# Narrower maxima, six score pieces, and the last two bodies' value products in three fp32r parts

## The reference

```
scores = q @ k.T / 8 - max(cum_i - cum_j, 0)        # cum: running sum of max(s, 0)
attn   = softmax(causal scores)                     # row maximum subtracted
x      = attn @ v, heads side by side               # (4, 576, 512)
h      = relu(x @ w_in); gate = sigmoid(conv3(h)); x1 = (h * gate) @ w_out
u      = x1 + (x1.T @ U @ V).T                      # U: 576 x 32, V: 32 x 576
out    = u + relu(u @ w_ch1) @ w_ch2
```

## Time and profile before

| | |
|---|---|
| median of 3 runs (884.1 to 886.88) | 885.18 us |
| profiled execution | 886.38 us |
| its span, first to last instruction | 884.6 us |
| PE (TensorE) busy | 853.1 us, 96% |
| DVE (VectorE) busy | 463.5 us, 52% |
| ACT (ScalarE) busy | 380.8 us, 43% |
| share of TensorE in the chain that ended last | 80% |
| mean granted TensorE clock | 0.998 |

### The profile page before, as it was taken

The page is one execution under the profiler, slowest core; times in us unless marked ns, Lnnn a source line. Parts: engine busy times, 40 slices in busy tenths (PEclk is TensorE's granted clock), DMA queues, the critical chain, the costliest instruction groups (busy, mean ns, idle before and its releaser), DMA issues.

```text
span 884.6 us, 15745 instructions
## 1 busy us (share of the span) xinstructions
PE 853.1 (96%) x6184; PEld 805.3 (91%) x6184; DVE 463.5 (52%) x976; ACT 380.8 (43%) x717; POOL 50.6 (6%) x106
## 2 busy tenths in 40 slices
PE   4988999989999999999999999999999999999998
PEld 3766889879998999999999999999999999999998
DVE  6787794565547825563445942555323832442222
ACT  3777674663436535553325642544213722121110
POOL 3021000000000000010000000000000000000000
PEclk9999999999999999999999999999999999999999
DMA  5574736726744346444444436325335443364541
GB/s 125 139 188 118 274 107 209 250 59 217 242 159 172 117 156 225 164 140 160 169 158 142 144 106 221 117 83 194 141 128 194 147 160 129 140 236 152 181 153 54
DMA packets 61837, 140.92 MB, mean 159 GB/s; under 512 B 29515, under 2 KB 43851, under 8 KB 49221
## 3 DMA queue, kind: packets, MB, share of 16 engines
q1 hardware_dynamic: 58692, 135.06, 45.7%
q0 software_dynamic: 3072, 4.87, 2.1%
HBM read 109.71 MB, written 30.11 MB: 158 GB/s over the span
## 4 chain that ended last, share of the span: by engine, by line
PE 80%; DVE 7%; issue 4%; ACT 4%; DMA 2%; SPq 1%; POOL 0%; DVEq 0%; ACTq 0%; POOLq 0%
PE psum L1256 22%; PE psum L1258 21%; PE psum L1257 21%; PE psum L1235 7%; PE psum L1180 2%; PE psum L1213 2%; PE psum L1211 2%; DVE work L1018 1%; DVE psum L959 1%; DVE work L1021 1%; PE psum L1193 1%; DMA few_scratch<-few 1%; PE psum L1322 1%; PE psum L1218 1%; ACT work L794 1%
## 5 line engine op out<-in xcount | busy, mean ns | idle before, releaser
L1256 PE MATMUL psum<-uu_hl,ring 128*128 128x288 f32 x512 | 152.9, 299 | 1.8 <-DVE uu_hl L1056 1.2
L1256 PE MATMUL psum<-r_hl,ring 128*128 128x288 f32 x512 | 152.9, 299 | 0.0
L1258 PE MATMUL psum<-r_hl,ring 128*128 128x288 f32 x512 | 151.2, 295 | 0.0
L1257 PE MATMUL psum<-r_hl,ring 128*128 128x288 f32 x512 | 151.1, 295 | 0.0
L1258 PE MATMUL psum<-uu_hl,ring 128*128 128x288 f32 x512 | 150.9, 295 | 0.0
L1257 PE MATMUL psum<-uu_hl,ring 128*128 128x288 f32 x512 | 150.8, 294 | 0.0
L838 ACT ACTIVATE r_hl<-psum 128x288 fp32r<-128x288 f32 x128 | 52.5, 411 | 187.9 <-PE psum L1258 187.8
L1061 DVE SCALAR_TENSOR_TENSOR r_hl<-psum,r_hl 128x288 fp32r<-128x288 f32 x128 | 58.3, 458 | 136.3 <-ACT r_hl L838 136.3
L959 DVE CUSTOM_DVE_ANT_0 psum<-psum,key_late 128x512 f32<-128x512 f32 (+4 forms) x160 | 84.3, 563 | 54.9 <-PE psum L1180 54.7
L1235 PE MATMUL psum<-probs,va 128*65 128x320 f32 (+4 forms) x448 | 109.3, 364 | 3.3 <-ACT probs L733 3.1
L1073 DVE TENSOR_TENSOR u_acc<-psum,u_acc 128x288 f32<-128x288 f32 x96 | 43.7, 457 | 116.2 <-PE psum L1258 116.2
(11 more groups left out here) (103 smaller groups left out, 1621.3 us busy)
## 6 DMA issues: line engine op xcount, KB each, us to landing
ring<-w_scratch SPq DMA_DIRECT2D x74, 1024.0 KB, 4.9
w_scratch<-ring SPq DMA_DIRECT2D x24, 1024.0 KB, 5.9
kq_raw<-in_kq_t SPq DMA_DIRECT2D x32, 288.0 KB, 4.1
stage<-in_w_ch SPq DMA_DIRECT2D x16, 512.0 KB, 5.8
spread_out<-few_scratch POOLq DMA_DIRECT2D x32, 144.0 KB, 3.1
out_t<-u_acc SPq DMA_DIRECT2D x16, 288.0 KB, 3.6
va<-in_v SPq DMA_DIRECT2D x32, 128.0 KB, 2.7
stage<-in_w_out SPq DMA_DIRECT2D x4, 512.0 KB, 5.1
```

The costliest lines, as they stand in the source:

```text
L1256: pe.matmul(o, hi, m_hi, start=start, stop=False)
L1257: pe.matmul(o, hi, m_lo, start=False, stop=False)
L1258: return pe.matmul(o, lo, m_hi, start=False, stop=stop)
```

## The change

- Tiles of query rows are laid from the end: tile 0 has rows 0 to 63, tile t rows 64 + 128 (t - 1) onwards. The widths of the maxima are 64, 192, 320, 448 and 576 instead of 128, 256, 384, 512 and 576. The rounds are {3, 0}, {2, 1}, {4}.
- Key tile 4 has its own 64 rows only, and the pieces of the scores are (1, 128, 576); (2, 256, 576); (0, 256, 576), (3, 384, 576); (0, 0, 256), (4, 512, 576). Each chunk has a mask product. Value products still end at query 256 where their PSUM bank does.
- U is loaded 96 columns wide instead of 128; the small loads come two steps earlier; V's low part is made a step later. The fp32 identity becomes the fp32r one.
- In bodies 2 and 3 (n >= `PARTED` = 16) ScalarE makes each chunk's exponentials twice, as the high part in one fp32r buffer and as fp32, and the values' high part (`values_high`) at step 0; VectorE makes both low parts; TensorE multiplies high x high and high x low values at step c + 1, and low probabilities x high values in `then` of step c + 1. Exponentials of chunk c are in step c, ahead of its items. The heads' evictions there are in `then` of step 4 except for head 7.

```diff
-    CHUNKS = [[(1, SPLIT, S)],
-              [(2, SPLIT, S)],
-              [(0, SPLIT, S), (3, 3 * P, S)],
-              [(4, 4 * P, S), (1, P, SPLIT), (0, 0, SPLIT)]]
+    CHUNKS = [[(1, P, S, 0)],
+              [(2, SPLIT, S, 0)],
+              [(0, SPLIT, S, 0), (3, 3 * P, S, S - SPLIT)],
+              [(0, 0, SPLIT, P // 2), (4, 4 * P, S, 0)]]
-        ROUNDS = [[3], [2, 0], [1, 4]]
+        ROUNDS = [[3, 0], [2, 1], [4]]
-        SMALL_AT = {(0, 4): 0, (1, 4): 1, (2, 2): 2}
+        SMALL_AT = {(0, 4): 0, (1, 2): 1, (2, 0): 2}
+        PARTED = 2 * H
+        def low_behind(h, c):
+            return h < H - 1 or c < NC - 1
+        def chunk_before(n, c, by):
+            m, at = divmod((n - PARTED) * NC + c - by, NC)
+            return (m, at + 1) if m >= 0 else None
...
-                      if any(x[0] in ("turn", "rank", "mix") for x in PLAN[a][GROUPS * h + GROUPS - 1])}
+                      if any(x[0] in ("turn", "rank", "mix") for x in PLAN[a][GROUPS * h + GROUPS - 1]) or a * H + h >= PARTED}
...
+                def exponentials_parted(a, h, c):
+                    n = a * H + h
+                    mm_s.wait(act, n, c + 1)
+                    if chunk_before(n, c, 1):
+                        mm_hi.wait(act, *chunk_before(n, c, 1))
+                        pl_done.wait(act, *chunk_before(n, c, 1))
+                    act.activation(probs_hl[0][:, 0:WIDTH[c]], psum[:, c % 2, 0:WIDTH[c]], ACT.Exp).then_inc(exps.sem, 1)
...
+                    act.activation(probs[:, c % 2, 0:WIDTH[c]], psum[:, c % 2, 0:WIDTH[c]], ACT.Exp).then_inc(whole.sem, 1)
+                def values_high(a, h):
...
+                    act.activation(va_hl[:, :, 0:D], va[i][:, :, 0:D], ACT.Copy).then_inc(vh_done.sem, 1)
...
                     if STEP_BEFORE.get((a, h, g)):
                         follow(STEP_BEFORE[a, h, g][-1])
+                    if a * H + h >= PARTED and g < NC:
+                        exponentials_parted(a, h, g)
...
+                def probabilities_low(a, h, c):
+                    n = a * H + h
+                    whole.wait(dve, n - PARTED, c + 1)
+                    mm_pv.wait(dve, n, c) if c else mm_pv.wait(dve, n - 1)
...
                 def then(a, h, g):
+                    if g < NC and a * H + h >= PARTED:
+                        probabilities_low(a, h, g)
...
+                    value_products(n, c, [(va_hl[:, :, 0:D + 1], probs_hl[0], True),
+                                          (va_hl[:, :, VLOW:VLOW + D], probs_hl[0], False)]).then_inc(mm_hi.sem, 1)
+                def values_of_low(a, h, c):
+                    n = a * H + h
+                    pl_done.wait(pe, n - PARTED, c + 1)
+                    value_products(n, c, [(va_hl[:, :, 0:D + 1], probs_hl[1], False)]).then_inc(mm_pv.sem, 1)
...
+                def then(a, h, g):
+                    if g >= 1 and a * H + h >= PARTED and low_behind(h, g - 1):
+                        values_of_low(a, h, g - 1)
```

More of the change, by code:

```diff
@@ L501, in load_v @@
                         return
-                    mm_pv.wait(sp, n - 2)
+                    mm_pv.wait(sp, n - 2) if n - 2 < PARTED else vl_done.wait(sp, n - 2 - PARTED)
                     of = v[source(a, h)]
@@ L1178, in max_scores @@
                             if r == 2 and n and bank not in started:
-                                red.wait(pe, n, 1 if bank == MX // BANK else 3)
-                            mm = pe.matmul(psf[:, at + j:at + e], qc[n % KCS][0:CROWS, q0:q0 + P], kc[n % KCS][0:CROWS, j:e],
+                                red.wait(pe, n, len(ROUNDS[0]) if bank == MX // BANK else len(ROUNDS[0] + ROUNDS[1]))
+                            mm = pe.matmul(psf[0:rows, at + j:at + e], qc[n % KCS][0:CROWS, q0:q0 + rows], kc[n % KCS][0:CROWS, j:e],
                                            start=bank not in started, stop=True, skip_group_check=True)
@@ L1216, in scores @@
[L1216 to L1220 removed]
+                    if chunk_before(n, c, 2):
+                        whole.wait(pe, *chunk_before(n, c, 2))
+                    for x, (t, i0, i1, at) in enumerate(CHUNKS[c]):
+                        k0, rows = t * P, key_rows(t)
+                        o = psum[0:rows, c % 2, at:at + i1 - i0]
+                        pe.matmul(o, kb[i][:, k0:k0 + rows], qb[i][:, i0:i1], start=(x == 0), stop=False,
+                                  skip_group_check=True)
+                        pe.matmul(o, kc[n % KCS][:, k0:k0 + rows], qc[n % KCS][:, i0:i1], start=False, stop=True,
+                                  skip_group_check=True)
@@ new lines, in scores, with value_products @@
+                    at, m0, m1 = LATE_AT[c]
+                    mm = pe.matmul(psum[:, c % 2, at:at + m1 - m0], ident_b[:, :], key_late_t[:, m0:m1],
+                                   start=False, stop=True, skip_group_check=True)
+                    mm.then_inc(mm_s.sem, 1)
+                def value_products(n, c, passes):
+                    out = out_at(n)
+                    for t, i0, i1, at in CHUNKS[c]:
+                        for j0, j1 in ((max(i0, SPLIT), i1), (i0, min(i1, SPLIT))):
+                            if j0 >= j1:
+                                continue
+                            rows, w0 = key_rows(t), at + j0 - i0
+                            for values, of, first in passes:
+                                values = values[0:rows, t, :]
+                                mm = pe.matmul(psf[0:values.shape[-1], out + j0:out + j1], values, of[0:rows, w0:w0 + j1 - j0],
+                                               start=first and t == 1, stop=True, skip_group_check=True)
+                    return mm
@@ L1246, in attention_step @@
                         values(a, h, g - 1)
+                        if a * H + h >= PARTED and not low_behind(h, g - 1):
+                            values_of_low(a, h, g - 1)
                     if g == turn_at(a, h) and a:
@@ L1384, in _ @@
                 pe.wait_ge(s_uvl, 2)
-                bodies(attention_step, ffn_step)
+                bodies(attention_step, ffn_step, then)
                 for item in END:
```

139 lines of the change are left out of this document (81 added, 58 removed).

## The result

After the change the kernel takes 905.2 us (median of 5 runs, 903.47 to 909.04), before it, on the same chip, 884.1 us (883.1 to 886.88): a ratio of 1.0236, 95% interval 1.0217 to 1.0255. The forecast was 896 us with a range of 883 to 905: the direction and the mechanism of the largest term came, the size was short by 9 us, and the median stands at the upper end of the range, 0.2 above it. The profiled run took 909.04 us, the slowest of the five, with a span of 907.2, 22.6 more than the span before (884.6).

A forecast was written before the change was run, and what follows sets the result against it. TensorE was taken to bound the kernel (busy 96% of the span), with VectorE also full in the wi stretches. Terms -2.2 - 1.6 - 2.0 + 1.0 + 15.4 = +10.6 on 886.4 gave 897.0, as a median 896 us, range 883 to 905.

The forecast's parts named there:

- the largest term: TensorE's new waits in the wi stretches of bodies 2 and 3: +15.4 us for the two.
- The handshake: Wi stretches, bodies 2 and 3: ScalarE's high probabilities wait for VectorE's previous difference, behind its FFN items; TensorE waits, +15.4 us.
- The walk through body 3: Body 3's wi stretch, followed operation by operation at measured durations: TensorE waits 8.1 us together, +7.7 over before.
- the first wait of the walk: Body 3, step (0,4): TensorE waits 2.2 us, with the head's eviction now behind the gate that waits for convolution 2.
- The price of the pieces: TensorE's score pieces, maxima, row transposes and fp32 values in every head: -0.07 us a head, -2.2 us for 32.
- Three products against fp32: Value products of heads 16 to 31: three fp32r products cost 0.10 us a head less than fp32, -1.6 us.
- rival 2: The three products stream at 0.42 ns a column, loads hidden, waits come too: 9.1 less, 887 us; chance 0.12.
- Body 0: Attention alone before 79.6 us: earlier loads shrink head 4's wait to about 1.0 us; -2.0 us, bounds -4 and +1.
- (1), the cover holds: Added VectorE and ScalarE work stays hidden and TensorE's saving comes out: median 882 us; chance 0.16.
- (3), the handshake in all steps: The handshake also stops turn, mix and wo steps, 18 a body with 0.3 us each: +11, 907 us; chance 0.10.

The follow-up runs named there:

- e3: The changed kernel with two buffers for the high probabilities instead of one: 892.98 us.
- e4: The kernel before, with the value product of key tile 4 cut to the 64 rows that hold values: 889.83 us.
- e2: The changed kernel with the value products of key tile 4 over 128 rows instead of 64: 901.08 us.
- e6: The changed kernel with fp32 values in all bodies, and key tile 4's value products and the row transposes over 128 rows: 882.62 us.
- e7: e6 with VectorE's first normalisation in body 0 two steps later: 879.59 us.
- e10: The changed kernel with only body 0's first normalisation moved two steps later: 900.09 us.
- e1: The changed kernel without its three products, all bodies keeping fp32 values; pieces, maxima, U and loads as changed: 886.85 us.
- e8: The changed kernel with two high buffers, 128 rows in values and transposes, and the first normalisation two steps later: 884.01 us.

## Why the prediction was right, and where it was short

*The handshake: right, place by place.* The walk through body 3 gave waits of 2.2, 1.4, 0.6, 0.4, 2.8 and 0.7 us; the trace has 1.53, 0.79, 0.65, 0.35, 2.37 and 0.99, with one of 0.46 at 489.12 that I did not have. Body 2 has 7.8 us of them, body 3 7.1; less the 1.46 and 0.40 of before that is +13.0, forecast +15.4. (0.46 us in each body, for `r_hl`, and 0.20 in body 2 are waits of another kind.) The times agree better still: the stretch begins 11.5 us late, and with that taken off, chunk 0's difference ends at 500.5 (walk: 500.4), chunk 2's at 515.0 (515.0), and the L840 behind it at 516.2 (516.2). That the sum was too high because TensorE, with its dearer products, came later to the same places is argued and not shown. e3 shows the cause of most of it: one buffer more, and 12.2 us are back. That the first wait of the walk comes from the later eviction was not tested by itself; e3 still has 4.3 us of waits for `va_hl`.

*The price of the pieces: the step that failed.* I had -0.07 us a head for them; the medians of the blocks over a head are 6.21 us before and 6.52 after, +0.31. Its parts: the score blocks came as priced (step 0 1.27 us, forecast 1.26; step 1 1.64 and 1.64), but the step-4 values take 0.88, where 320 columns by my prices make about 0.61, and the row transposes 1.40 where they took 1.22. I priced an instruction by its columns and by whether a load of 128 columns follows, took the values' columns as unchanged and so their cost as unchanged, and did not ask about the rows, though `key_rows(t)` is in the diff. The rows of before have 97 rows next to 128, and none with 64; this cost was never bounded. e4 puts it into the kernel before (some +5 us), e2 and e6 take it out (-4.1, -4.2). With 128 rows everywhere (e7) a head's blocks take 6.05 us, 0.16 less than before, forecast 0.07 less: without the rows the price was right in direction and 0.1 us from it in size. In time the +0.31 shows in bodies 2 and 3; in body 1 heads 10 to 15 together take 0.2 us more than before.

*Three products against fp32: right in size by luck.* Forecast -0.10 us a head; as changed -0.11 (6.42 against 6.52), with 128 rows -0.30. The forecast knew nothing of the rows, so the -0.30 is what it should have had: a saving sized too small by 0.2 us and a row cost that is paid twice a head here and once in fp32 cancel. The price of the long products was right: 320 columns follow each other at 0.147 us, as 0.46 ns a column makes, and not at the 0.133 of rival 2. That rival had 10.7 us in all; with full rows it is 4.8.

*Body 0: the second term that failed, -2.0.* The wait of head 4 shrank to less than I said (0.35, forecast about 1), and head 4 gained 3.2 us, forecast 2.8. But I asked only what the earlier loads take away and not what VectorE meets next: the normalisation's DMA. The whole body gained 0.7 us, forecast 2.6 with its share of the pieces, and even that is no gain of the change: head 0 alone is 2.4 us shorter, as it is in e4's trace with the old order of pieces, and in both the clock rises some 6 us earlier than in the trace before. Heads 1 to 7 take 54.5 us, before 52.6. e10 gives 5.1 us for moving that operation in the changed kernel (heads 1 to 7: 49.0), e7 3.0 in the other.

*Does it add up?* 905.2 less e2's 4.1 and e10's 5.1 is 896.0, the forecast; e1 less the gains of e6 and e7 is 879.6, where the forecast for the pieces was 880. So the two causes have the size of what was missed in both versions of the kernel, 9 us in the first and 7 in the second. That it closes so well is luck in part: each of the four differences is uncertain by about 2 us, e2 leaves the transposes' 64 rows in, and the waits came 2.4 us under their forecast, which nothing in this sum makes up for.

*The rivals.* (1), the cover holds, is refuted by the waits. (3), the handshake in all steps, gave 907, near the measured time, for the wrong reason: heads 19 to 23 and 27 to 30, outside the wi stretches, take between 0.1 us less and 0.9 us more than before (0.3 on average, forecast 0.1 to 0.2 less), of which 0.2 are the rows; 6 to 10 us a body do not lie there. A time alone would have spoken for it.

*What stays open:* why 64 rows lay a load bare and 66, 96 and 97 do not; why the DMA of a normalisation lands in time in one execution and not in another; and, of e8 over e7, the last 1.2 us by the medians, 2.4 by the traces.

## What to carry to other kernels

When a ring of engines hands one buffer around (here exponential, difference, exponential), find what else stands in each one's program between its turns, and walk one round at measured durations: here that gave all but one of the waits, each to within 0.7 us, and one more buffer took most of it away. A half-empty tile costs TensorE nothing as zeros, and a quarter of a microsecond each time if the operand is cut to 64 rows between full ones, so look at the number of rows, not only at the columns, and measure a number that no row of yours shows. Where an edit ends a wait, look at the next operation on the engine that was late: if it depends on a DMA that was hidden by the old wait, the time goes there.

## What the runs showed of the hardware that was not expected

**A change between 64 rows and more lays the weight load bare.** Between products with 128 rows each, a load starts one product ahead (437.78 for 437.91). The load with 64 rows started at 438.11, when the product before it had passed, and the next 128-row one at 438.29 likewise. Cost: 0.285 us for each such pair of changes in the kernel before (e4), 0.26 to 0.29 in fp32 step 4 (0.884 against 0.599), 0.23 in the three products (0.38 against 0.15). It does not matter which half is used: e4 takes the upper 64 rows, the changed kernel the lower. Other numbers of rows show nothing of it. In the changed kernel the loads from 128 to 96 rows, from 96 to 128 and from 66 to 128 start 0.003 us (median) behind the start of the product before, those from 128 to 97 rows 0.05 behind it; those from 128 to 64 rows start 0.2 to 0.3 behind it and those from 64 to 128 0.15, each within 0.002 us of its own product. The load of the bf16 mask product, too, starts with its product (438.80 for 438.81), with 128 rows; that case was not followed.

The Trainium skill, page "TensorE: Matmul & The Clock Gate", section "The mechanism", says that a load overlaps running products only if it goes to other row groups. The trace does not agree: the loads to the same 128 rows are hidden, and those to or from 64 rows are not. The text of that section also has a load pulled ahead if it targets a background weight buffer, which would fit the 128-row loads; no run here shows which buffer a load takes.

**A wait can cost more than its length.** In the changed kernel the granted clock falls to the lower level (1.2 GHz) just before TensorE resumes after its 4.01 us wait at 57.04, and stays there for 6.8 us (56.3 to 63.1); in body 3 it does so just before the end of the 2.37 us wait, for 3.4 us (527.3 to 530.7). It does not follow each time: the 2.37 us wait of body 2, which ends at 305.98, has no low clock behind it, and the stretch of 6.8 us from 87.0 on comes after waits of 1.08 and 0.21 us. Windows of the changed kernel, and below them the same two of e7, where head 5 does not wait; columns as above, the clock is the third number from the end:

```profile
50.00:60.00 10.00, 5.99 (x28) 4.10 (x28) 6.78 (x17) 4.08 (x8) 0.56 (x1) 0.81 0.36 99
60.00:70.00 10.00, 10.00 (x58) 6.50 (x57) 8.12 (x19) 7.60 (x13) 2.32 (x4) 0.85 0.47 129
```

```profile
50.00:60.00 10.00, 9.14 (x61) 6.45 (x59) 9.22 (x22) 8.48 (x14) 2.33 (x4) 1.00 0.51 131
60.00:70.00 10.00, 9.09 (x63) 6.56 (x61) 8.86 (x27) 8.50 (x16) 1.09 (x2) 1.00 0.78 182
```

A TensorE that shows 10.00 of 10 busy at a clock of 0.85 is not at its peak: the busy share does not show what the clock takes.
